# Token-interleaved row tiles in a linear-attention and mixture kernel: strided stationary operand, three output rows per store packet

## The reference

```python
# 1. gated linear attention; B, H, S, D = 4, 8, 768, 48
f = 1 / (1 + exp(-f_logit))
for t in range(S):
    state = f[:, :, t, :, None] * state + k[:, :, t] (outer) v[:, :, t]
    y[:, :, t] = q[:, :, t] @ state
x = y.transpose(0, 2, 1, 3).reshape(B * S, H * D)        # 3072 tokens x 384

# 2. dense mixture of E = 4 experts, F = 1024
p = domain_probs / (domain_probs.sum(-1, keepdims=True) + 1e-9)
for e in range(E):
    out += p[:, e:e+1] * (relu(x @ w1[e]) @ w2[e])

# 3. soft mixture: 8 experts with 4 slots each (32 slots)
logits = out @ phi
d = column softmax of logits;  c = row softmax of logits
slot_out = per-expert MLP of (d.T @ out)                 # weights v1, v2
return c @ slot_out                                      # 3072 x 384
```

## Time and profile before

| | us |
|---|---|
| median of 3 runs | 1021.33 |
| lowest and highest | 1019.85, 1021.47 |
| the profiled execution, device time | 1019.76 |
| its span, first to last instruction | 1018.0 |
| its granted TensorE clock, mean share of full | 0.996 |
| TensorE matmuls busy | 1000.3 (98%) |
| DVE, ACT, POOL busy | 355.9, 289.2, 123.4 |

### The profile page before, as it was taken

One profiled execution on the slowest core, in us unless ns is written; L12 is line 12 of the kernel. 1 busy time (PEld: TensorE's weight loads), 2 busy tenths in 40 slices (PEclk: granted clock), 3 DMA queues, 4 the chain that ended last, 5 costly groups with the idle time before them and its releaser, 6 DMA issues.

```text
span 1018.0 us, 18033 instructions
## 1 busy us (share of the span) xinstructions
PE 1000.3 (98%) x7044; PEld 949.3 (93%) x7044; DVE 355.9 (35%) x776; ACT 289.2 (28%) x609; POOL 123.4 (12%) x147
## 2 busy tenths in 40 slices
PE   8999999999999999999999999999999999999994
PEld 7899999999999999999999999999999999999842
DVE  6565646546543222222222222222222222222333
ACT  5553443343323311111133111111322222222322
POOL 3541221122101400000023000000320000000000
PEclk9999999999999999999999999999999999999998
DMA  9763333432303200000003000000030004011785
GB/s 189 187 113 63 66 78 65 88 71 57 75 17 132 94 32 0 0 0 0 1 1 124 0 0 0 0 0 0 0 124 1 1 1 186 0 62 63 248 311 186
DMA packets 131122, 67.05 MB, mean 66 GB/s; under 512 B 106864, under 2 KB 126832, under 8 KB 131056
## 3 DMA queue, kind: packets, MB, share of 16 engines
q1 hardware_dynamic: 126416, 63.87, 22.7%
q10 hardware_dynamic: 4640, 2.31, 0.8%
HBM read 56.72 MB, written 4.72 MB: 60 GB/s over the span
## 4 chain that ended last, share of the span: by engine, by line
PE 91%; SPq 4%; DVE 2%; DMA 1%; issue 1%; ACT 0%; DVEq 0%
PE ph L1674 13%; PE po L1693 13%; PE po L1695 13%; PE po L1694 13%; PE ph L1676 13%; PE ph L1675 13%; PE pair L1622 2%; PE pc L1650 2%; PE pc L1656 1%; PE ph L1911 1%; PE pair L1632 1%; PE po L1926 1%; SPq L723 1%; PE pair L1755 1%; PE pair L1604 1%; SPq L749 1%
## 5 line engine op out<-in xcount | busy, mean ns | idle before, releaser
L1287 DVE SCALAR_TENSOR_TENSOR h_lo<-ph,h_hi 128x384 fp32r<-128x384 f32 x256 | 142.5, 557 | 503.7 <-ACT h_hi L1012 502.6
L1012 ACT ACTIVATE h_hi<-ph 128x384 fp32r<-128x384 f32 x256 | 126.0, 492 | 510.1 <-PE ph L1676 510.1
L1674 PE MATMUL ph<-xT,w_hi 128*128 128x384 f32 (+1 forms) x768 | 263.6, 343 | 0.1
L1693 PE MATMUL po<-w_hi,h_hi 128*128 128x384 f32 x768 | 259.9, 338 | 0.1
L1676 PE MATMUL ph<-xT,w_lo 128*128 128x384 f32 (+1 forms) x768 | 257.2, 335 | 0.0
L1695 PE MATMUL po<-w_hi,h_lo 128*128 128x384 f32 x768 | 257.0, 335 | 0.0
L1675 PE MATMUL ph<-xT,w_hi 128*128 128x384 f32 (+1 forms) x768 | 257.0, 335 | 0.0
L1694 PE MATMUL po<-w_lo,h_hi 128*128 128x384 f32 x768 | 256.7, 334 | 0.0
L1674 PEld LDWEIGHTS ph<-xT,w_hi 128*128 128x128 f32 x768 | 144.2, 188 | 8.2 <-issue 7.8
L1693 PEld LDWEIGHTS po<-w_hi,h_hi 128*128 128x128 f32 x768 | 144.2, 188 | 2.3 <-issue 1.5
L1675 PEld LDWEIGHTS ph<-xT,w_hi 128*128 128x128 f32 x768 | 144.4, 188 | 0.0
(11 more groups left out here) (279 smaller groups left out, 758.0 us busy)
## 6 DMA issues: line engine op xcount, KB each, us to landing
v<-in_moe_w_dram SPq DMA_DIRECT2D x12, 1536.0 KB, 9.0
raw<-in_moe_w_dram SPq DMA_DIRECT2D x6, 1536.0 KB, 8.7
q_in<-in_q_dram SPq DMA_DIRECT2D x48, 96.0 KB, 2.6
v_in<-in_v_dram SPq DMA_DIRECT2D x48, 96.0 KB, 2.6
k_in<-in_k_dram SPq DMA_DIRECT2D x47, 96.0 KB, 2.6
f_in<-in_f_logit_dram SPq DMA_DIRECT2D x43, 96.0 KB, 2.6
out_dram<-out_sb SPq DMA_DIRECT2D x5, 768.0 KB, 6.0
x_raw<-yT SPq DMA_DIRECT2D x46, 72.0 KB, 2.2
```

The source lines that it names most:

```text
L1012: a.activation(h_hi[:, f % 2, :], ph[f % 2][:, 0:BLK], ACT.Relu).then_inc(h_hi_done, 1)
L1287: d.scalar_tensor_tensor(out=h_lo[:, f % 2, :], in0=ph[f % 2][:, 0:BLK], scalar=0.0, in1=h_hi[:, f % 2, :].bitcast(F32), op0=ALU.max, op1= ...
L1674: t.matmul(bank, wh, xh, start=(kk == 0), stop=False, skip_group_check=True)
L1693: t.matmul(bank, hh, w2_hi[:, f, :], start=(f == 0), stop=False, skip_group_check=True)
```

## The change

Tile s of half n now holds the tokens 384 n + 3 p + s. The second product takes every third column of `h_hi` and `h_lo` as its stationary operand, 12 bytes apart, where it took 128 adjacent ones. All that works by rows later (`x2`, the logits, the softmaxes, `x2T`) goes by tile and partition as before; only `dp` and `out` name memory rows, and both get the new map. The tokens of a partition's three tiles are adjacent rows of `out`, so the stores can take three rows, 4608 bytes, in a run, and the runs of `dp` become 48 bytes. The groups of the stores change to (0, 2), (2, 3), (3, 6), (6, 12), (12, 18), (18, 24).

```diff
-        out_dram = out.rearrange("(i p) d -> p i d", p=P)
+        out_dram = out.rearrange("(n p s) d -> p n s d", p=P, s=BT)
@@
-        OUT_TILES = [(0, 2)] + [(i, min(i + 4, NT)) for i in range(2, NT, 4)]
+        OUT_TILES = [(0, 2), (2, 3), (3, 6)] + [(i, i + 2 * BT) for i in range(6, NT, 2 * BT)]
@@
-                    sp.dma_start(dp[:], probs.rearrange("(i p) e -> p i e", p=P)).then_inc(small_in, 16)
+                    sp.dma_start(dp[:].rearrange("p (n s) e -> p n s e", s=BT),
+                                 probs.rearrange("(n p s) e -> p n s e", p=P, s=BT)).then_inc(small_in, 16)
@@
             for i0, i1 in OUT_TILES:
-                sp.wait_ge(act_out, i1 // 2)
+                sp.wait_ge(act_out, (i1 + 1) // 2)
                 sp.wait_ge(dve_out, i1 // 2)
-                sp.dma_start(out_dram[:, i0:i1, :], out_sb[:, i0:i1, :]).then_inc(out_done, 16)
+                n, s0 = divmod(i0, BT)
+                if i1 - i0 > BT:
+                    sp.dma_start(out_dram[:, n:i1 // BT].rearrange("p n s d -> p n (s d)"),
+                                 out_sb[:, i0:i1, :].rearrange("p (n s) d -> p n (s d)", s=BT)).then_inc(out_done, 16)
+                else:
+                    sp.dma_start(out_dram[:, n, s0:s0 + i1 - i0], out_sb[:, i0:i1, :]).then_inc(out_done, 16)
@@
-                hh, hl = h_hi[:, f % 2, s * P:(s + 1) * P], h_lo[:, f % 2, s * P:(s + 1) * P]
+                hh = h_hi[:, f % 2].rearrange("p (a s) -> p s a", s=BT)[:, s]
+                hl = h_lo[:, f % 2].rearrange("p (a s) -> p s a", s=BT)[:, s]
```

## The result

The changed kernel takes 1034.24 us, the median of 4 runs (1033.26 to 1034.79), where the kernel before takes 1020.64 us beside it (1019.85 to 1021.47). The ratio is 1.0128, 95% interval [1.0116, 1.014]: 1.3% slower. The forecast of 1019.5 us and its range to 1022.5 both missed.

What follows compares the result with a forecast made beforehand. TensorE, busy 1000.3 of 1018.0 us, was taken to bound the kernel by its stream's pace and few standstills. Strided loads nothing, stores 1.28 plus dp 0.56 made 1.84 us less: 1021.33 to 1019.5 us, range 1018.0 to 1022.5.

Steps and rivals of the forecast that it cites:

- Strided operand: Second product's 2304 weight loads, address step 4 to 12 bytes: no cost, hidden behind the 173.4 ns product.
- the doubling: A strided weight load taking twice 110 ns: 46.6 ns for each of 2304 products, 107 us.
- rival (a): L1693 to L1695, all stage 2: strided read paces weight loads from k (load time over 110 ns) = 1.58; chance 0.18.
- The bound of "nothing": Second product's weight loads: no cost if the load's pace stays below 173.4 ns; no gain either.
- The rule of the Trainium skill: Strided weight loads: 16-byte SBUF lines need two hits for full bandwidth; k = 1.5, estimated 165 ns a load.
- Stores: Output stage: 4608-byte runs raise 364 GB/s to 407; data take 11.68 us instead of 12.96, 1.28 us less.
- The price per packet: Output stores: 0.037 ns a byte from 4096- and 1536-byte loads, so a 4608-byte store packet takes 181 ns.
- No pause: Output stage: coarser store groups would not starve the stream near 1006.8, with 0.4 us to spare.
- Rival (b): Output stage: stores go no faster, only dp's 0.56 us is left, 1020.8 us; chance 0.20.
- Load of dp: Stage 1: 3072 runs become 1024, phi_sb's issue shortens up to 1.39 us, TensorE's 0.56 us wait for kd goes.
- rival (c): Stores and dp both reach upper bounds, 1.43 + 1.39 = 2.82 us less, 1018.5 us; chance 0.14.
- Sum: Whole kernel: stores 1.28 + dp 0.56 = 1.84 us less, median 1021.33 to 1019.5.

Runs made afterwards that it cites:

- wide_strided: Kernel before with 512 moving columns in the second product for f = 0 to 6 and its stationary operand 12 bytes apart: 1151.77 us.
- step_8_bytes: Kernel before with the 2304 stationary operands of the second product read 8 bytes apart: 1024.5 us, one run.
- low_first_tile_8_bytes: Kernel before with only h_lo of tile 0 read 8 bytes apart, one weight load in a step (256 loads): 1026.16 us, one run.
- stride_only: Kernel before with nothing changed but the strided (12-byte) stationary operand of the second product: 1036.44 us, ratio 1.0151.
- maps_only: Changed kernel with the packed stationary operand of before; maps of dp and out and store groups stay changed: 1018.31 us against 1021.22, ratio 0.9977.
- order_in_h: Changed kernel with packed weight loads, token order made where h_hi and h_lo are written: 1019.14 us (ratio 0.9986), second series 1018.71 us (0.9981).
- order_in_xT: Changed kernel with packed weight loads, token order made when ScalarE and VectorE write xT: 1020.58 us, ratio 0.9998.
- low_first_tile: Kernel before with the 12-byte strided operand for h_lo of tile 0 alone, one load in 18 (256 loads): 1029.24 us, one run.
- all_8_bytes: Kernel before with the stationary operands of both products read 8 bytes apart, 4608 loads: 1020.74 us, one run, beside 1019.6 before.
- wide_packed: Kernel before with 512 instead of 384 moving columns in the second product for f = 0 to 6, loads packed: 1140.33 us, one run.

## Why the prediction was wrong, point by point

**Strided operand: the step that failed.** "I take nothing, as the nearest row (110 ns, packed) leaves 58% for a slower read; the doubling is a rival." The load's length was within the bound: it grew by 64 ns, and (110 + 64) / 110 = 1.58, the very point from which rival (a) was to decide (at 16 bytes the same sum, 110 + 143 = 253 ns, lies above the measured pace of 233, so it gives rather too much). But "It is hidden up to k = 173.4 / 110 = 1.58" took for granted that a load which ends in time costs nothing. Two things speak against it. With 231 ns at its disposal the 12-byte load still cost its product 3.6 ns (wide_strided), and the 8-byte load, 6 ns longer and free of cost where all are alike, cost 25 ns a step where it stood among packed ones (step_8_bytes, low_first_tile_8_bytes). The bound of "nothing" was right for the first term only at 8 bytes, and the second was in no bound at all. In the steps of stage 2 the term that was taken as nothing measured 59 ns, 32 in the strided products and 27 in the packed ones behind them; over the whole kernel it measured 15.2 us by medians and 15.9 by VectorE's first eviction (stride_only).

**Rival (a)** named the right place and the right sign, with 0.18. Its price was wrong: 44 us at k = 1.75, 107 at 2, nothing up to 1.58, where some 15 us came at k = 1.58. Of its signs one came (the pace of the strided products above 173.4) and one did not: hidden() with unchanged loads slowed down as well. The range left (a) out; with a price for small k it would have had to reach some 1035.

**The rule of the Trainium skill** ("SBUF — State Buffer", Specifications) had been read as two slots for each 16-byte line, an estimated 165 ns. The same reading gives 188 ns in the records for 8 bytes, and 194 were measured; for 12 bytes 188 + 55 = 243 against 252 measured; for 16 bytes 188 + 110 = 298 against 331. So the trace agrees that two words in a line are nearly free and that the cost starts beyond; the sizes are larger, and the measurement decides. I weighed the rule against the wrong limit, the length of the product.

**Stores: right.** Forecast 407 GB/s and 11.68 us of data, measured 405 and 11.66; gain 1.28 forecast, 1.26 measured from the twelfth eviction to the end. The price per packet, taken from loads of two packet sizes, carried over to stores. No pause showed near the third group. Rival (b) is out.

**Load of dp: right.** phi_sb's issue fell by 1.25 us, and TensorE's 0.56 us wait for kd went in every kernel with the new load. The start of a turn alone doesn't show the gain, since executions reach the turn ahead of dp's at different times (55.52 us before, 55.85 in maps_only, 55.54 and 56.97 in the two of order_in_h). The time from that turn to the one after dp's wait does: 10.75 us before and 10.11 or 10.12 in all four kernels with the new load and packed operands (maps_only, order_in_xT and both of order_in_h). That is 0.6 us where 0.56 was forecast. From there to the last turn of stage 1 before takes 231.59 us, maps_only 231.63 and order_in_h 231.62: nothing more is gained, and rival (c), that the later loads carry 1.39 us on, is out.

**Sum.** Without the strided loads the forecast would have been 1019.5, and maps_only is at 1018.31 and the two series of order_in_h at 1019.14 and 1018.71. Against the kernel before beside them these are 2.9, 1.2 and 1.7 us less, where 1.84 was forecast. The mechanism and the sizes of the gains held; one term of 15 us, taken as nothing, turned the sign.

## What to carry to other kernels

An operation that fits into the time of the one it hides behind is not yet free: on a TensorE stream that is busy 98% of the time, 4 ns in half of the products, or one odd weight load in 18, is up to a per cent of the kernel (9 us of 1020 in low_first_tile). Before a stream of thousands of equal instructions is touched, give its smallest disturbance a price per instruction and multiply, and let the range reach there. If an order of rows is wanted for larger packets, make it on an engine with slack and in PSUM reads, as order_in_h does, and keep the stationary operands packed and all of one kind.

## What the runs showed of the hardware that was not expected

- An fp32r weight load of 128 columns is recorded with 188 ns packed, 194 at 8 bytes, 252 at 12 and 331 at 16. The products of 384 columns follow at 173.4, 173.4 and 177.9 ns where all loads of a step are alike, and at 233 in the half of a step that has 16-byte loads.
- The 12-byte load costs 3.6 to 4.4 ns of the product whether the product lasts 173 or 231 ns. What the two share I can't say from the records.
- Packed loads that follow on 8-byte or 12-byte ones, and products of 384 columns that follow on those of 512, lose some 20 to 38 ns in a step, spread over the next five to eight products, even if the load differed by only 6 ns; going to 8-byte loads or to the wider product costs nothing that the averages show. In step_8_bytes nothing else starts or ends in those five products in the timeline, and the granted clock (0.994 to 0.997 in all runs profiled) is that of the kernel before. What it is inside TensorE stays open; that it comes with the change and not with the strided load is shown by all_8_bytes, for 8 bytes.
- A product of 512 columns takes 231 ns in wide_packed, one of 384 takes 173.3: in proportion to the columns, 0.451 ns each.
- ScalarE reads SBUF 12 bytes apart in 716 ns where it takes 514 packed (384 columns), 0.53 ns more for each; the weight load's 64 ns are 0.50 for each of 128. Reading PSUM 12 bytes apart costs neither ScalarE nor VectorE anything (492 and 557 ns).
